# Strided attention and two split-precision MLPs on one core: the attention's end and the MLPs' beginning in another order, and the softmax's constant added on VectorE

## The chip, the cores and the metric

The kernel runs on one core of a Trainium2 chip. The metric is device time in microseconds (us); lower is better. TensorE multiplies matrices, VectorE and ScalarE work on tiles in SBUF and PSUM, GpSimd on tiles in SBUF, and SyncE issues the DMAs. In the profile they are called PE (PEld for the weight loads), DVE, ACT, POOL and SP.

## The reference

Attention over 2 x 8 heads of 576 tokens with 64 channels, each head with one of two masks, then an MLP with squared ReLU (512 to 2048 to 512), then four experts (512 to 1024 to 512) whose outputs are summed with normalised shares.

```python
scores = scale * np.matmul(q, k.transpose(0, 1, 3, 2))
scores = np.where(masks[None, :, :, :], scores, -1000000000.0)   # local: last 32; strided: same pos % 32
scores = scores - np.max(scores, axis=-1, keepdims=True)
attn = np.exp(scores)
attn = attn / (np.sum(attn, axis=-1, keepdims=True) + 1e-09)
x = np.matmul(attn, v)                       # then laid out as 1152 tokens x 512
h = np.maximum(x @ w_in, 0.0)
x = h * h @ w_out
for e in range(4):
    out += p[:, e:e + 1] * (np.maximum(x @ w1[e], 0.0) @ w2[e])
```

## The kernel before

**Attention.** It goes over eight pairs of heads n (0 to 7; 0, 1, 4, 5 are local, the others strided). For a pair TensorE computes the scores (L1065), VectorE adds the mask and takes the row extreme (`scores_max`, L725), ScalarE exponentiates block by block and accumulates the row sums in the same instruction (`exps`, L548), ScalarE adds 1e-9 to the sums (L554), VectorE takes the reciprocal (`recip`, L735), GpSimd multiplies (L493), TensorE transposes (L1085), VectorE copies the transposes out (`pT_copy`, L742), TensorE multiplies by v (`outputs`, L1111), and ScalarE or VectorE copies the result out (`att_out`). `warm_up` (L1119) are matmuls whose result nobody reads.

**MLPs.** A matrix product is split in two ways. Each float32 operand is split into a high and a low part, and three passes (L1122 to L1124) make one product. On top of it stands a seven-product scheme for 2 x 2 blocks (M1 to M7, computed in the order M1, M2, M6, M7, M4, M5, M3). Its input forms T1 to T4 are differences of blocks of x (`t_forms`, L770; `pair_forms` for the attention's end), S1 to S4 sums of weight blocks (`sums`, GpSimd). The high parts are made on ScalarE (`x_high`, `wa_high`, `wb_high`), the low parts on GpSimd (`x_low` L482, `wa_low` L442, `wb_low` L448). The combinations of the products are made by VectorE (`second_sum`, `third_sum`, `fourth_sum`, `c_block` L860) with a copy of M1 that ScalarE makes (`first_product`, L608). For the first MLP ScalarE takes the ReLU (`rectified`, L615), VectorE squares (`square`, L866), ScalarE writes `h_hi` (`h_high`, L622), VectorE writes `h_lo` (`h_low`, L873; L876 for the experts).

**Order.** The token halves and groups of 512 hidden units give 24 steps t. ORDER is A0, B0, A1, A2, B1, A3, B2, ... A7, B6, B7, A8, A9, B8, ...: "A t" computes the hidden block t (84 matmuls of the seven products), "B t" its share of the output (tiles of 12 matmuls). t below 8 is the first MLP; B's tiles alternate between two PSUM banks, and tile n waits until tile n - 2 is copied out (`y_copy` L600 on ScalarE for B0, `y_tile` L887 and L889 on VectorE from B1 on). Each engine runs its own list, written out by hand, strictly in that order; only semaphores tie the engines together. So the order in which an engine's code is written is the schedule. Block 0 starts inside the last pair of attention.

The waits of TensorE that matter below:

```python
elif k == M6:
    pe.wait_ge(s_m1, 2 * t + u + 1)
elif k == M7:
    pe.wait_ge(s_c, tile_count(t, C11, u))
...
if t == 0:
    pe.wait_ge(s_att, NP)
    pe.wait_ge(s_t[1], t_done(1, T4))
    pe.wait_ge(s_h_lo, tile_count(0, C21, 1))
```

In B0 the wait on `wb_lo` for the tile's own columns stands behind these, and the wait on all of block 0's `h_lo` stands at tile 4. In B8 the wait on all four `wb_lo` parts of the group stands behind the wait on `h_lo`.

Of the kernel before, what the change touches and what calls it, by code (L numbers as in the profile page):

```python
# [30 lines left out]
def attention_then_mlps(nc, qt, kt, v_near, v_far, wa, wb, probs, out):  # L31
# [57 lines left out]
    with ExitStack() as ctx:  # L89
# [71 lines left out]
        ssum = little("ssum", [P, 2, 2, 3, MAXB])  # L161
# [234 lines left out]
        def _(pool):  # L396
# [26 lines left out]
            nc.gpsimd.memset(ssum[:, :, :, :, :], 1.0).then_inc(s_stat_zero, 1)  # L423
# [62 lines left out]
            for n in range(NP):  # L486
# [3 lines left out]
                for h in range(2):  # L490
# [3 lines left out]
                        p_ap, p_ap, ssum[0:qw, n % 2, h, 2, 0:even].unsqueeze(2).to_broadcast([qw, even, kw]),  # L494
                        ALU.mult)
                    for i in range(even, nb):
# [3 lines left out]
                            p_ap, p_ap, ssum[0:qw_i, n % 2, h, 2, i:i + 1].to_broadcast([qw_i, kw_i]), ALU.mult)  # L500
# [21 lines left out]
            for kind, t in ORDER:  # L522
                s = t // 2
                if kind == "A" and t % 2 == 0 and 0 < t and s + 1 < SUBS:
                    sums(s + 1, S1, S3, S2, S4)
                if kind == "A" and t % 2 == 1:
# [3 lines left out]
                    if t == 1:  # L530
                        sums(1, S1, S3, S2, S4)
# [9 lines left out]
        def _(act):  # L541
            def exps(n, h, blocks):
                for i in blocks:
                    _, qw, _, kw, c0 = blocks_of(n)[i]
                    p_ap = prob[n % PROBS][0:qw, h, c0:c0 + kw]
                    if h == 0:
                        act.wait_ge(s_max, blocks_before(n) + i + 1)
                    ins = nc.scalar.activation(p_ap, p_ap, ACT.Exp, scale=-1.0, bias=smin[0:qw, n % 2, h, i:i + 1],  # L548
                                               accum_out=ssum[0:qw, n % 2, h, 0, i:i + 1])
                if i == len(blocks_of(n)) - 1:  # L550
                    ins.then_inc(s_exp, 1)
                    nb, qw = len(blocks_of(n)), blocks_of(n)[0][1]
# [63 lines left out]

            def h_high(t, q):
# [10 lines left out]
            act.wait_ge(s_stat_zero, 3)  # L628
# [17 lines left out]
            att_out(NP - 2)  # L646
            first_product(0)
            x_high(0, 3)
            x_high(0, 4)
# [23 lines left out]
            for k in (3, 4, 5, 6):  # L673
                x_high(1, k)
                y_copy(k + 1)
            for kind, t in ORDER[1:]:
                s = t // 2
                if kind == "B":
                    if t == BLOCKS1 - 2:
                        for k in range(FORMS):  # L680
                            x_high(2, k)
                    continue
                first_product(t)
                if t == 1:
                    for q in (C11, C21, C22, C12):
                        rectified(1, q)
                        if q != C12:
                            wa_high(1, 2 * q)
                        h_high(1, q)
                        if q != C12:  # L690
                            wa_high(1, 2 * q + 1)
                    wa_high(1, 6)
                    continue
# [3 lines left out]
                if t == BLOCKS1:  # L697
                    for k in range(FORMS):
                        x_high(3, k)
# [14 lines left out]
        def _(dve):  # L714
# [37 lines left out]
            def t_forms(i, *which):  # L752
                c = i % 2
                blocks, b12 = x_blocks(c)
                for k in which:
                    if i == 0:
                        dve.wait_ge(s_att, PAIRS)
                    else:
                        dve.wait_ge(s_y, y_tiles(BLOCKS1 - 4 + i) + (KT if k == T1 else 2 * KT))
# [10 lines left out]
                    nc.vector.tensor_tensor(t_form[:, c, k, :, :], a, b, ALU.subtract).then_inc(s_t[i], 1)  # L770

# [135 lines left out]
            dve.wait_ge(s_stat_zero, 3)  # L907
# [45 lines left out]
            for u in range(2):  # L953
                square(0, C22, u)
# [3 lines left out]
            for u in range(2):  # L958
                square(0, C12, u)
# [329 lines left out]
```

## Time and profile before

| | |
|---|---|
| three runs | 641.86, 642.80, 643.49 us (median 642.8) |
| the profiled execution | span 640.1 us, time 641.86 us |
| TensorE busy | 619.5 us (97%) |
| VectorE / ScalarE / GpSimd busy | 375.0 / 247.7 / 293.8 us |
| mean granted TensorE clock | 0.995 |

The profiled execution is the shortest of the three runs, 0.9 us below their median; between its span and its time lie 1.8 us. TensorE stands idle for 640.1 - 619.5 = 20.6 us of the span. A wait row names the releaser that the last wait instruction points to, which need not be the one that came last.

### The profile page before, as it was taken

What the parts mean: (1) busy time and instruction counts of PE and PEld (TensorE: products, weight loads), DVE (VectorE), ACT (ScalarE), POOL (GpSimd) and SP (SyncE); (2) the same over time, 40 slices, a digit from 0 to 9 for tenths busy, and PEclk for the clock granted to TensorE, in tenths of its full rate; (3) what the DMA queues carried; (4) which work ended last, traced back from release to release, by engine and by line L of the source; (5) the groups of instructions that cost most, each with busy time, mean ns of one, the idle gap of its engine ahead of it and who ended that gap; (6) DMA issues with size and microseconds to landing.
All of it is one profiled execution on the core that took longest, in us unless ns stands there. A gap on an engine that the chain in (4) does not pass through costs nothing.

```text
span 640.1 us, 11296 instructions
## 1 busy us (share of the span) xinstructions
PE 619.5 (97%) x4182; PEld 576.7 (90%) x4182; DVE 375.0 (59%) x980; ACT 247.7 (39%) x674; POOL 293.8 (46%) x249
## 2 busy tenths in 40 slices
PE   8879898999999999999999999999999999999998
PEld 7769897999999999989899899899899889889986
DVE  4876557585585586673564564564565465456452
ACT  6997655362362363461151151241241331232210
POOL 4987784255055058695065064074073173260200
PEclk9999998999999999999999999999999999999999
DMA  8440301012022012021011021011021022020012
GB/s 321 158 133 2 132 2 67 1 67 67 1 67 67 2 66 68 0 67 67 1 67 67 1 67 66 2 67 67 0 67 67 1 66 67 2 67 1 0 51 98
DMA packets 16486, 35.87 MB, mean 56 GB/s; under 512 B 2864, under 2 KB 3120, under 8 KB 16432
## 3 DMA queue, kind: packets, MB, share of 16 engines
q1 hardware_dynamic: 16432, 35.15, 16.4%
q8 instruction: 33, 0.54, 0.3%
q14 instruction: 21, 0.17, 0.1%
HBM read 32.79 MB, written 2.36 MB: 55 GB/s over the span
## 4 chain that ended last, share of the span: by engine, by line
PE 83%; DVE 7%; ACT 6%; issue 2%; POOL 2%; DVEq 0%; ACTq 0%; POOLq 0%
PE ps L1122 27%; PE ps L1124 26%; PE ps L1123 26%; ACT prob L548 3%; DVE h_lo L873 2%; DVE ps L860 1%; PE ps L1119 1%; DVE ps L866 1%; POOL xf_lo L482 1%; DVE prob L725 1%; PE ps L1065 1%; ACT xf_hi L595 1%; PE ps L1111 1%; ACT h_hi L622 1%; ACT wa_hi L572 1%
## 5 line engine op out<-in xcount | busy, mean ns | idle before, releaser
L1122 PE MATMUL ps<-xf_hi,wa_hi 128*128 128x288 f32 x672 | 200.4, 298 | 4.1 <-ACT m L608 3.7
L1123 PE MATMUL ps<-xf_lo,wa_hi 128*128 128x288 f32 x672 | 199.2, 296 | 0.0
L1124 PE MATMUL ps<-xf_hi,wa_lo 128*128 128x288 f32 x672 | 198.6, 296 | 0.0
L448 POOL TENSOR_TENSOR wb_lo<-raw_b,wb_hi 128x512 fp32r<-128x512 f32 x48 | 60.7, 1303 | 186.6 <-ACT wb_hi L581 186.6
L1122 PEld LDWEIGHTS ps<-xf_hi,wa_hi 128*128 128x128 f32 x672 | 127.0, 189 | 5.7 <-ACT wa_hi L572 3.5
L1123 PEld LDWEIGHTS ps<-xf_lo,wa_hi 128*128 128x128 f32 x672 | 126.9, 189 | 0.5
L1124 PEld LDWEIGHTS ps<-xf_hi,wa_lo 128*128 128x128 f32 x672 | 127.3, 189 | 0.0
L1122 PE MATMUL ps<-wb_hi,h_hi 128*128 128x512 f32 x288 | 112.3, 390 | 1.1 <-DVE h_lo L876 1.1
L1124 PE MATMUL ps<-wb_hi,h_lo 128*128 128x512 f32 x288 | 112.4, 390 | 0.0
L1123 PE MATMUL ps<-wb_lo,h_hi 128*128 128x512 f32 x288 | 112.4, 390 | 0.0
L903 DVE SCALAR_TENSOR_TENSOR y<-ps,p_norm,y 128x512 f32<-128x512 f32 (+1 forms) x64 | 47.4, 742 | 96.1 <-PE ps L1124 96.1
L625 ACT ACTIVATE h_hi<-ps 128x288 fp32r<-128x288 f32 x128 | 51.1, 410 | 106.6 <-DVE ps L860 106.6
L608 ACT ACTIVATE m<-ps 128x288 f32<-128x288 f32 x48 | 19.4, 412 | 182.9 <-PE ps L1124 182.9
L1122 PE MATMUL ps<-h_hi,wb_hi 128*128 128x288 f32 x256 | 76.5, 299 | 4.0 <-POOL wb_lo L448 1.6
L1124 PE MATMUL ps<-h_hi,wb_lo 128*128 128x288 f32 x256 | 75.5, 295 | 0.0
L1123 PE MATMUL ps<-h_lo,wb_hi 128*128 128x288 f32 x256 | 75.4, 295 | 0.0
L860 DVE TENSOR_TENSOR ps<-ps,u 128x288 f32<-128x288 f32 x144 | 66.9, 466 | 5.1 <-issue 0.4
L442 POOL TENSOR_TENSOR wa_lo<-raw_a,wa_hi 128x512 fp32r<-128x512 f32 x36 | 46.8, 1308 | 41.6 <-ACT wa_hi L572 41.6
L1122 PEld LDWEIGHTS ps<-wb_hi,h_hi 128*128 128x128 f32 x288 | 54.1, 188 | 12.1 <-DVE h_lo L876 1.3
L1124 PEld LDWEIGHTS ps<-wb_hi,h_lo 128*128 128x128 f32 x288 | 54.1, 188 | 11.4
L1123 PEld LDWEIGHTS ps<-wb_lo,h_hi 128*128 128x128 f32 x288 | 54.1, 188 | 10.9
L442 POOL TENSOR_TENSOR wa_lo<-s_form,wa_hi 128x512 fp32r<-128x512 f32 x48 | 61.1, 1293 | 5.2 <-ACT wa_hi L572 5.1
(77 smaller groups left out, 868.6 us busy)
## 6 DMA issues: line engine op xcount, KB each, us to landing
raw_a<-in_wa SPq DMA_DIRECT2D x48, 256.0 KB, 3.8
raw_b<-in_wb SPq DMA_DIRECT2D x24, 512.0 KB, 4.9
q_buf<-in_q SPq DMA_DIRECT2D x8, 288.0 KB, 4.7
k_buf<-in_k SPq DMA_DIRECT2D x8, 288.0 KB, 4.6
result<-y SPq DMA_DIRECT2D x8, 256.0 KB, 2.0
v_loc<-in_v_near SPq DMA_DIRECT2D x4, 384.0 KB, 4.6
v_str<-in_v_far SPq DMA_DIRECT2D x4, 320.0 KB, 5.5
result<-y SPq DMA_DIRECT2D x2, 128.0 KB, 1.8
```

The costliest lines, as they stand in the source:

```text
L442: nc.gpsimd.tensor_tensor(wa_lo[:, k, :, :], where[:, i, :, :], wa_hi[:, k, :, :].bitcast(F32), ALU.subtract).then_inc(s_wa_lo, 1)
L448: nc.gpsimd.tensor_tensor(wb_lo[:, :, cols], raw_b[:, :, cols], wb_hi[:, :, cols].bitcast(F32), ALU.subtract).then_inc(s_wb_lo, 1)
L482: nc.gpsimd.tensor_tensor(xf_lo[:, c, k, :, :], src, xf_hi[:, c, k, :, :].bitcast(F32), ALU.subtract).then_inc(s_xf_lo, 1)
L548: ins = nc.scalar.activation(p_ap, p_ap, ACT.Exp, scale=-1.0, bias=smin[0:qw, n % 2, h, i:i + 1], accum_out=ssum[0:qw, n % 2, h, 0, i:i + 1])
L608: nc.scalar.activation(m1[:, u, :], ps[:, bank(t, M1, u), 0:HT], ACT.Copy).then_inc(s_m1, 1)
L625: nc.scalar.activation(dst, src, ACT.Relu).then_inc(s_h_hi, 1)
L860: nc.vector.tensor_tensor(ps[:, hbank(t, q, u), 0:HT], ps[:, bank(t, k, u), 0:HT], other[:, u, :], ALU.add)\
L873: nc.vector.tensor_tensor(lo, ps[:, hbank(t, q, u), 0:HT], hi.bitcast(F32), ALU.subtract)\
L903: nc.vector.scalar_tensor_tensor(out=out_acc[:, i, d], in0=src, scalar=p_norm[:, i, e:e + 1], in1=out_acc[:, i, d], op0=ALU.mult, op1=ALU. ...
L1122: nc.tensor.matmul(dst, a_hi, b_hi, start=first, stop=False)
L1123: nc.tensor.matmul(dst, a_hi, b_lo, start=False, stop=False)
L1124: return nc.tensor.matmul(dst, a_lo, b_hi, start=False, stop=last)
```

## The change

**Softmax.** The 16 ScalarE instructions that add 1e-9 go. The accumulated sum and a constant 1e-9 now lie side by side (two more small memsets on GpSimd at the start), and VectorE sums the two with a `tensor_reduce` ahead of each reciprocal.

**End of attention.** TensorE computes M2 of block 0 in two halves with the outputs of pair 6 and the next transposes between them. ScalarE copies M1 and makes one x form ahead of `att_out` of pair 6.

**Block 0.** ScalarE takes over the squares of C22 and C12, and its list around them is reordered. **Block 1.** ScalarE copies M1 of block 2 ahead of the last `h_high`. **B blocks.** `y_tile` 1 moves between the two halves of C22. **Transition to the experts.** The forms T2 to T4 of sets 2 and 3 are made in halves inside B6 and B7, the high parts of set 3 are interleaved with `h_high` of block 8, and GpSimd makes the sums of group 5 behind `wb_low` of group 4.

```diff
-            return {T1: 1, T2: 2, T3: 3, T4: 4}[k]
+            return {T1: 1, T2: 5, T3: 6, T4: 7}[k]
...
-                if kind == "A" and t % 2 == 0 and 0 < t and s + 1 < SUBS:
+                if kind == "A" and t % 2 == 0 and t not in (0, BLOCKS1) and s + 1 < SUBS:
                     sums(s + 1, S1, S3, S2, S4)
                 if kind == "A" and t % 2 == 1:
                     if t > 1:
                         for d in range(KT):
                             wb_low(s, d)
-                    if t == 1:
-                        sums(1, S1, S3, S2, S4)
+                    if t in (1, BLOCKS1 + 1):
+                        sums(s + 1, S1, S3, S2, S4)
...
-                                               accum_out=ssum[0:qw, n % 2, h, 0, i:i + 1])
+                                               accum_out=ssum[0:qw, n % 2, h, i, 0:1])
                 if i == len(blocks_of(n)) - 1:
                     ins.then_inc(s_exp, 1)
-                    nb, qw = len(blocks_of(n)), blocks_of(n)[0][1]
-                    act.wait_ge(s_exp, 2 * n + h + 1)
-                    nc.scalar.activation(ssum[0:qw, n % 2, h, 1, 0:nb], ssum[0:qw, n % 2, h, 0, 0:nb], ACT.Copy,
-                                         bias=1e-9).then_inc(s_sum, 1)
...
+            def squared(t, q):
+                for u in range(2):
+                    act.wait_ge(s_relu, tile_count(t, q, u))
+                    nc.scalar.activation(ps[:, hbank(t, q, u), 0:HT], relu[:, u, :], ACT.Square).then_inc(s_sq, 1)
...
-            att_out(NP - 2)
             first_product(0)
             x_high(0, 3)
+            att_out(NP - 2)
...
             x_high(1, 0)
             rectified(0, C22)
+            squared(0, C22)
+            h_high(0, C22)
             y_copy(0)
             x_high(1, 1)
-            h_high(0, C22)
+            rectified(0, C12)
+            squared(0, C12)
+            h_high(0, C12)
             y_copy(1)
-            rectified(0, C12)
             x_high(1, 2)
-            y_copy(2)
-            h_high(0, C12)
-            y_copy(3)
...
+                    rectified(1, C12)
+                    first_product(2)
+                    h_high(1, C12)
                     wa_high(1, 6)
...
             def recip(n, h):
                 nb, qw = len(blocks_of(n)), blocks_of(n)[0][1]
+                dve.wait_ge(s_exp, 2 * n + h + 1)
+                nc.vector.tensor_reduce(srec[0:qw, n % 2, h, 0, 0:nb], ssum[0:qw, n % 2, h, 0:nb, :], AX.X, ALU.add)\
+                    .then_inc(s_sum, 1)
                 dve.wait_ge(s_sum, 2 * n + h + 1)
...
+            def half_forms(i, kt):
...
+                dve.wait_ge(s_y, y_tiles(BLOCKS1 - 4 + i) + KT + 2 * (kt + 1))
+                for k in (T2, T3, T4):
...
+                    nc.vector.tensor_tensor(t_form[:, c, k, kt, :], a[:, kt, :], b[:, kt, :], ALU.subtract)\
+                        .then_inc(s_t[i], 1)
...
-                            if i == 0:
-                                for u in range(2):
-                                    h_low(follows[1], C22, u)
-                                    c_block(follows[1], C12, u)
+                            if i < 2:
+                                h_low(follows[1], C22, i)
+                                c_block(follows[1], C12, i)
...
+                        if t >= BLOCKS1 - 2 and i == KT - 1:
+                            t_forms(t - BLOCKS1 + 4, T1)
+                        if t >= BLOCKS1 - 2 and i in (KT + 1, KT + 3):
+                            half_forms(t - BLOCKS1 + 4, (i - KT) // 2)
...
                 if n == NP - 1:
-                    product(0, M2)
+                    product(0, M2, [0])
...
             prob_transposes(NP - 1, 0)
+            product(0, M2, [1])
             product(0, M6, [0])
```

Three places in the engines' order. ScalarE at the end of block 1, where `relu`, `h_hi`, `wa_hi` and `m` are the outputs of `rectified`, `h_high`, `wa_high` and `first_product`; before:

```order
L572 ACTIVATE wa_hi<-s_form 128x512
L615 ACTIVATE relu<-ps 128x288 x2
L572 ACTIVATE wa_hi<-raw_a 128x512
L622 ACTIVATE h_hi<-ps 128x288 x2
L572 ACTIVATE wa_hi<-s_form 128x512
L615 ACTIVATE relu<-ps 128x288 x2
L622 ACTIVATE h_hi<-ps 128x288 x2
L572 ACTIVATE wa_hi<-s_form 128x512
L608 ACTIVATE m_62<-ps 128x288 x2
```

and after, where the copy of M1 (`m`) stands ahead of the last `h_hi`:

```order
L573 ACTIVATE wa_hi<-s_form 128x512
L616 ACTIVATE relu<-ps 128x288 x2
L573 ACTIVATE wa_hi<-raw_a 128x512
L628 ACTIVATE h_hi<-ps 128x288 x2
L573 ACTIVATE wa_hi<-s_form 128x512
L616 ACTIVATE relu<-ps 128x288 x2
L609 ACTIVATE m_62<-ps 128x288 x2
L628 ACTIVATE h_hi<-ps 128x288 x2
L573 ACTIVATE wa_hi<-s_form 128x512
```

The copy moved forward past one pair of `h_hi` and one `wa_hi`.

VectorE in B1, where `y` is `y_tile`, `h_lo` and `ps<-ps,u` are `h_low` and `c_block` of the block computed ahead of it; before:

```order
L887 COPY y<-ps 128x288
L873 TENSOR_TENSOR h_lo<-ps,h_hi 128x288
L860 TENSOR_TENSOR ps<-ps,u_63 128x288
L873 TENSOR_TENSOR h_lo<-ps,h_hi 128x288
L860 TENSOR_TENSOR ps<-ps,u_63 128x288
L887 COPY y<-ps 128x288
L866 SCALAR_TENSOR_TENSOR ps<-ps,relu 128x288 x2
L887 COPY y<-ps 128x288
L873 TENSOR_TENSOR h_lo<-ps,h_hi 128x288 x2
```

and after:

```order
L929 COPY y<-ps 128x288
L915 TENSOR_TENSOR h_lo<-ps,h_hi 128x288
L902 TENSOR_TENSOR ps<-ps,u_63 128x288
L929 COPY y<-ps 128x288
L915 TENSOR_TENSOR h_lo<-ps,h_hi 128x288
L902 TENSOR_TENSOR ps<-ps,u_63 128x288
L908 SCALAR_TENSOR_TENSOR ps<-ps,relu 128x288 x2
L929 COPY y<-ps 128x288
L915 TENSOR_TENSOR h_lo<-ps,h_hi 128x288 x2
```

The second `y` moved forward past one `h_lo` and one `c_block`; nothing else moved.

GpSimd at the transition, where `xf_lo` are the low parts of x sets 2 and 3, `s_form` the sums of group 5 and `wb_lo` the low parts of group 4; before:

```order
L482 TENSOR_TENSOR xf_lo<-t_form,xf_hi 128x576 x4
L482 TENSOR_TENSOR xf_lo<-y,xf_hi 128x576
L458 TENSOR_TENSOR s_form<-raw_a 128x512
L460 TENSOR_TENSOR s_form<-raw_a 128x512
L464 TENSOR_TENSOR s_form<-s_form,raw_a 128x512
L468 TENSOR_TENSOR s_form<-raw_a,s_form 128x512
L448 TENSOR_TENSOR wb_lo<-raw_b,wb_hi 128x4x128 x4
L442 TENSOR_TENSOR wa_lo<-raw_a,wa_hi 128x512 x2
```

and after:

```order
L487 TENSOR_TENSOR xf_lo<-y,xf_hi 128x576 x3
L487 TENSOR_TENSOR xf_lo<-t_form,xf_hi 128x576 x4
L487 TENSOR_TENSOR xf_lo<-y,xf_hi 128x576
L453 TENSOR_TENSOR wb_lo<-raw_b,wb_hi 128x4x128 x4
L463 TENSOR_TENSOR s_form<-raw_a 128x512
L465 TENSOR_TENSOR s_form<-raw_a 128x512
L469 TENSOR_TENSOR s_form<-s_form,raw_a 128x512
L473 TENSOR_TENSOR s_form<-raw_a,s_form 128x512
L447 TENSOR_TENSOR wa_lo<-raw_a,wa_hi 128x512 x2
```

The four `wb_lo` moved ahead of the four `s_form`.

## Rows read from the trace of the kernel before

**Rows 1.** Windows: length, PE, PEld, DVE, ACT, POOL busy (instructions), clock, DMA share, GB/s.
```profile
20.00:45.00 25.00, 20.74 (x257) 17.96 (x258) 20.29 (x125) 24.72 (x115) 22.39 (x22) 1.00 0.56 173
...
46.70:50.10 3.40, 3.40 (x32) 3.18 (x29) 1.19 (x5) 2.84 (x12) 3.07 (x3) 0.50 0.02 5
84.00:94.00 10.00, 10.00 (x77) 10.00 (x77) 6.51 (x16) 4.85 (x11) 8.65 (x8) 1.00 0.00 1
101.30:104.70 3.40, 3.40 (x16) 3.40 (x16) 1.65 (x5) 0.77 (x2) 0.67 (x1) 0.50 0.42 133
264.00:290.00 26.00, 24.53 (x161) 22.80 (x160) 19.41 (x45) 14.75 (x33) 24.49 (x20) 1.00 0.13 42
290.00:600.00 310.00, 310.00 (x1817) 281.29 (x1816) 166.67 (x346) 85.52 (x196) 115.89 (x92) 1.00 0.13 42
```

**Rows 2.** Waits of TensorE, whole run: waiter, named releaser, us in total, times, longest.
```profile
PE ps L1122 <- ACT m L608: 3.7, 2, 3.1
...
PE ps L1119 <- DVE probT L742: 2.1, 1, 2.1
...
PE ps L1122 <- POOL wb_lo L448: 1.6, 1, 1.6
PE ps L1122 <- DVE y L889: 1.2, 5, 0.3
PE ps L1122 <- DVE h_lo L876: 1.1, 1, 1.1
```

**Rows 3.** TensorE in order of time: start, length, instruction, idle before it and named releaser.
```profile
69.14 0.37 PE L1122 MATMUL ps<-h_hi,wb_hi 128*128 128x288 f32 x1 [1.59 <-POOL wb_lo L448]
...
76.66 0.40 PE L1122 MATMUL ps<-h_hi,wb_hi 128*128 128x288 f32 x1 [0.96 <-DVE h_lo L873]
...
97.36 0.29 PE L1122 MATMUL ps<-xf_hi,wa_hi 128*128 128x288 f32 x1
...
101.06 0.37 PE L1122 MATMUL ps<-xf_hi,wa_hi 128*128 128x288 f32 x1 [3.15 <-ACT m L608]
...
139.49 0.30 PE L1122 MATMUL ps<-h_hi,wb_hi 128*128 128x288 f32 x1
...
140.31 0.40 PE L1122 MATMUL ps<-h_hi,wb_hi 128*128 128x288 f32 x1 [0.26 <-DVE y L889]
...
281.77 0.29 PE L1122 MATMUL ps<-xf_hi,wa_hi 128*128 128x288 f32 x1
...
283.42 0.47 PE L1122 MATMUL ps<-wb_hi,h_hi 128*128 128x512 f32 x1 [1.09 <-DVE h_lo L876]
```

**Rows 4.** The small operations of lines 554 and 807: ns min/median/max, starts.
```profile
L554 ACT ACTIVATE ssum<-ssum x16: 206/208/209, 9.8 to 53.0; 96x6 f32<-96x6 f32 x8, 126x5 f32<-126x5 f32 x8
...
L807 DVE TENSOR_REDUCE p_sum<-p_raw x1: 180/180/180, 124.4 to 124.4; 128x9 f32<-128x36 f32 x1
```

**Rows 5.** VectorE in order of time, places of the first two MLP blocks and before.
```profile
41.89 0.18 DVE L735 RECIPROCAL ssum<-ssum 96x6 f32<-96x6 f32 x1 [1.36 <-ACT ssum L554]
...
68.48 0.45 DVE L873 TENSOR_TENSOR h_lo<-ps,h_hi 128x288 fp32r<-128x288 f32 x1
...
139.80 0.45 DVE L889 TENSOR_TENSOR y<-ps,y 128x288 f32<-128x288 f32 x1
```

**Rows 6.** ScalarE in order of time, blocks 0 and 1 of the first MLP.
```profile
69.46 0.41 ACT L615 ACTIVATE relu<-ps 128x288 f32<-128x288 f32 x1 [0.45 <-DVE ps L860]
...
71.00 0.41 ACT L600 ACTIVATE y<-ps 128x288 f32<-128x288 f32 x1 [1.13 <-PE ps L1124]
...
98.39 0.70 ACT L615 ACTIVATE relu<-ps 128x288 f32<-128x288 f32 x2
...
100.51 0.70 ACT L608 ACTIVATE m<-ps 128x288 f32<-128x288 f32 x2
```

**Rows 7.** GpSimd in order of time, ahead of the first expert block's output.
```profile
278.12 5.04 POOL L448 TENSOR_TENSOR wb_lo<-raw_b,wb_hi 128x512 fp32r<-128x512 f32 x4
```

**Rows 8.** Line 770, differences of two SBUF tiles: ns min/median/max, starts.
```profile
L770 DVE TENSOR_TENSOR t_form<-y x5: 719/1067/1394, 46.8 to 264.3; 128x576 f32<-128x576 f32 x5
```

More of the change, by code:

```diff
@@ L663, in _ @@
             rectified(0, C22)
+            squared(0, C22)
+            h_high(0, C22)
             y_copy(0)
             x_high(1, 1)
-            h_high(0, C22)
+            rectified(0, C12)
+            squared(0, C12)
+            h_high(0, C12)
             y_copy(1)
-            rectified(0, C12)
             x_high(1, 2)
-            y_copy(2)
-            h_high(0, C12)
-            y_copy(3)
-            for k in (3, 4, 5, 6):
-                x_high(1, k)
-                y_copy(k + 1)
+            for k in (2, 3, 4, 5):
+                y_copy(k)
+                x_high(1, k + 1)
+            y_copy(6)
+            y_copy(7)
             for kind, t in ORDER[1:]:
@@ L681, in _ @@
                             x_high(2, k)
+                    if t == BLOCKS1 - 1:
+                        x_high(3, 0)
                     continue
-                first_product(t)
+                if t != 2:
+                    first_product(t)
                 if t == 1:
-                    for q in (C11, C21, C22, C12):
+                    for q in (C11, C21, C22):
                         rectified(1, q)
-                        if q != C12:
-                            wa_high(1, 2 * q)
+                        wa_high(1, 2 * q)
                         h_high(1, q)
-                        if q != C12:
-                            wa_high(1, 2 * q + 1)
+                        wa_high(1, 2 * q + 1)
+                    rectified(1, C12)
+                    first_product(2)
+                    h_high(1, C12)
                     wa_high(1, 6)
+                    continue
+                if t == BLOCKS1:
+                    x_high(3, 1)
+                    x_high(3, 2)
+                    h_high(t, C11)
+                    x_high(3, 3)
+                    h_high(t, C21)
+                    x_high(3, 4)
+                    x_high(3, 5)
+                    h_high(t, C22)
+                    x_high(3, 6)
+                    h_high(t, C12)
                     continue
@@ L770, in t_forms @@
                     nc.vector.tensor_tensor(t_form[:, c, k, :, :], a, b, ALU.subtract).then_inc(s_t[i], 1)
+            def half_forms(i, kt):
+                c = i % 2
+                blocks, b12 = x_blocks(c)
+                dve.wait_ge(s_y, y_tiles(BLOCKS1 - 4 + i) + KT + 2 * (kt + 1))
+                for k in (T2, T3, T4):
+                    if k == T2:
+                        dve.wait_ge(s_t[i], 1)
+                        a, b = blocks[B22], t_form[:, c, T1, :, :]
+                    elif k == T3:
+                        a, b = blocks[B22], b12
+                    else:
+                        dve.wait_ge(s_t[i], 3 * kt + 2)
+                        a, b = blocks[B21], t_form[:, c, T2, :, :]
+                    nc.vector.tensor_tensor(t_form[:, c, k, kt, :], a[:, kt, :], b[:, kt, :], ALU.subtract)\
+                        .then_inc(s_t[i], 1)
             def pair_t1(n):
@@ L971, in _ @@
                         second_sum(t, u)
-                    if t == BLOCKS1:
-                        t_forms(3, T3, T4)
                     if moe1(t):
```

36 lines of the change are left out of this document (11 added, 25 removed).

## Prediction

> **What bounds the kernel now.** I read the windows first. From 290 to 600 us TensorE is busy for all 310.00 us; in 264 to 290 us it is busy for 24.53 of 26.00 us [rows 1]. So the experts' steady part has nothing to give, and the change, which touches only what lies before about 290 us, can only work on TensorE's gaps there. The list of TensorE's waits names them: 3.7 us for the copy of M1 (3.1 of it in one wait), 1.6 for `wb_lo`, 1.2 in five waits for `y`, 1.1 for `h_lo` (L876), and 2.1 once for `probT` in attention [rows 2]. Then I went to each place in TensorE's order of time. Three passes of a 128x288 product stand 0.40 us apart where nothing is waited for (77 matmuls in 10.00 us, some records missing [rows 1]), so what a wait costs is the start after it less the start before it, less 0.40. This slip is larger than the idle time in the row. It is 101.06 - 97.36 - 0.40 = 3.30 us for M6 of block 2, 140.31 - 139.49 - 0.40 = 0.42 for tile 3 of a B block, 283.42 - 281.77 - 0.40 = 1.25 at the start of B8 [rows 3].
>
> Two names mislead. At 69.14 the row names `wb_lo` [rows 3], but the wait that counts is that on `h_lo` of C21 ahead of it: VectorE wrote it at 68.48 and ended at 68.93 [rows 5]. At 283.42 the row names `h_lo` [rows 3], but four `wb_lo` run from 278.12 for 5.04 us, to 283.16 [rows 7]. I take these two as the releasers, because TensorE starts 0.2 to 0.3 us behind them.
>
> The clock is the last view. TensorE was granted half of its full clock (1.2 for 2.4 GHz) from 46.7 to 50.1 us and from 101.3 to 104.7, full clock in the other windows read [rows 1]. The second fall comes just as the 3.15 us wait ends at 101.06; in it TensorE did 16 matmuls in 3.40 us against 3.40 / 0.133 = 25.5 at full clock, which is 9.5 x 0.133 = 1.3 us lost, and 1.5 by the ratio of the clocks less the first few passes. I take 1.4.
>
> **The change, part by part.** *Constant on VectorE.* It removes 16 ScalarE instructions of 0.208 us [rows 4], 3.3 us. In 20 to 45 us ScalarE is busy for 24.72 of 25.00 us, VectorE for 20.29, GpSimd for 22.39 [rows 1]. The early ones gain nothing, since `att_out` of the first pairs waits for TensorE's outputs. From pair 3 on ScalarE leads until the reciprocal at 41.89, for which VectorE stood idle for 1.36 us [rows 5]. Five of the removed instructions lie in that stretch: 5 x 0.21 = 1.05 us. The added `tensor_reduce` isn't in the trace in this shape; the nearest row is that of line 807 with 0.18 us [rows 4], and about 0.07 for the wait of the reciprocal on it, so I take 0.25 each. Ahead of the reciprocal it stands in for ScalarE's instruction. But VectorE works in order, and behind the reduce of pair 6 waits a `pT_copy` for which TensorE waits: +0.25. Bounds for a reduce: nothing (the wait hidden) and 0.5 (a reduce as long as VectorE's 128x288 work, 0.45 [rows 5]). Sum -0.8, bounds -1.3 and +0.5. The two memsets end before the first scores arrive. This costs nothing unless the first ones grow by microseconds.
>
> *M2 in halves, M1's copy earlier.* No matmul is added. M6 waited 3.7 - 3.1 = 0.6 us for M1's copy [rows 2], which stood behind `att_out` of pair 6; now the copy comes first and half of M2 covers the rest: -0.6, bounds -0.9 and 0. GpSimd gets its x forms some 2 us earlier. That hides, but buys nothing: B0's start is set by VectorE's `h_lo` of C21, and VectorE's list up to it is untouched. So the wait at 69.14 stays, only shifted.
>
> *Squares on ScalarE in block 0.* ScalarE's list around the `y_copy` of 71.00 changes, before which it stood idle for 1.13 us [rows 6]. I lay its new list out from the second ReLU of C22 at 69.46, with 0.31 from start to start for two 128x288 of the same kind (a pair takes 0.70, one 0.41 [rows 6]): squares at 69.8 and 70.1, `h_hi` at 70.4 and 70.7, `y_copy` 0 at 71.0, x form at 71.3, ReLUs of C12 at 71.9 and 72.7 (behind VectorE's two `c_block`), squares 73.0 and 73.3, `h_hi` 73.6 and 73.9, `y_copy` 1 at 74.2 to 74.6. Tile 4's wait for `h_lo`, 0.96 idle at 76.66 [rows 3] and 1.1 as slip, goes. In its place tile 3, which would start at 69.14 + 3 x 1.6 = 73.9, waits for `y_copy` 1 until 74.7: 0.8. Net -0.3, bounds -1.1 (the squares quicker) and +0.5 (each square dearer by 0.2). If `Square` needed another activation table, loads would be added; the built list has one table load, as before.
>
> *M1's copy of block 2.* Before, the two ReLUs of C12 stand at 98.39 and the two copies at 100.51, with TensorE released at 101.06 by the first of them, 0.55 after its start [rows 3, 6]. Now the copies follow the ReLUs: first one at 98.39 + 2 x 0.31 = 99.0, TensorE at 99.55, 1.5 us earlier. Behind the copies wait `h_hi` and `h_lo` of C12 and then the `c_block` for which M7 waits; it comes at about 101.25 and M7 would want to start at 99.55 + 1.6 = 101.15, so 0.25 of it is given back. -1.25, bounds -1.5 and -0.8. What is left of the gap is 1.8 us. The wait of 1.59 at 69.14 [rows 3] is as long and lies between dense matmuls as well, and the clock did not fall behind it. So I count the fall as gone: -1.4, bound 0.
>
> *`y_tile` 1 earlier in B1 to B6.* Before, the copy at 139.80 ended at 140.25 and TensorE went on at 140.31 [rows 3, 5]. Moved ahead of one `h_low` and one `c_block`, it ends some 0.85 us earlier, and the slip of 0.42 goes. But `c_block` of the second half comes 0.37 later, and ReLU, square and `y_tile` 2 follow it; tile 4 then waits about 0.14. Six blocks x 0.28 = -1.7; bounds -2.5 (six whole slips) and -0.6.
>
> *Transition.* Without the two `t_forms` in the middle of block 8, VectorE no longer holds up M3 of block 8 and M1 of block 9: idle 24.53 against 26.00 us [rows 1] is 1.47, of which 1.09 is the wait at 283.42 [rows 3], so 0.4 here, some 0.7 as slip. GpSimd makes `wb_lo` ahead of four sums of 1.3 us, and the slip of 1.25 at 283.42 goes. -1.95. What is queued behind: the sums then end about where `wa_lo` began before, 283.1, and block 10 has five tiles of B8 to wait for. The half forms cost VectorE more in B6 and B7. Line 770 with two tiles of x took 0.72 to 1.39 us for 576 columns [rows 8]. Three halves at 0.4 to 0.75 and their waits are 1.4 to 2.5 us between `y_tile` 5 and 6; up to 2.3 the tiles hide it, above that tile 0 of B7 waits: bounds -1.95 and -1.3.
>
> On those 1.39 us the Trainium skill, "SBUF — State Buffer", on the shared port pair, says that a VectorE instruction with two SBUF inputs contends with a GpSimd instruction that reads SBUF, and the second to issue blocks until the first has finished. By that rule a half form beside GpSimd's 1.3 us work would wait for it whole: three forms near 3 us, a stall of some 0.6 at B7's tile 0. The trace bears out that the same form takes twice the time at some places, not which of the two waits.
>
> Sum: 0.8 + 0.6 + 0.3 + 1.25 + 1.4 + 1.7 + 1.95 = 8.0 us. On the profiled execution's own 641.86 that gives 633.9. It was the shortest of the three, 0.9 below the median, so a median of the changed kernel may stand as much above its best; I take 634.4.
>
> **Rivals.** (1) *The clock still falls behind the remaining 1.8 us.* For it: in attention it fell after a shorter wait, the 2.1 us for `probT` [rows 2], though among short matmuls. 634.4 + 1.4 = 635.8. (2) *Attention gains more.* VectorE and ScalarE being shorter, the wait of 2.1 us for `probT` [rows 2] shrinks to about 1.3, and the fall at 46.7 [rows 1] goes: 634.4 - 1.5 = 632.9. (3) *VectorE becomes attention's bound and ScalarE's new list stalls B0.* VectorE has 25.00 - 20.29 = 4.7 us of idle time, but in small waits on TensorE; the reduces take 9 x 0.25 = 2.3 of it. Then the first and third terms are lost: 635.5 to 637. (4) *Slower.* A single mechanism: the reduce and the wait on it. There are 16, in order, ahead of `pT_copy` and `scores_max`. If each cost p, attention would grow by 16 x (p - 0.25) once VectorE's slack is used, and the whole becomes slower than 642.8 + 1.9 where that exceeds 10.3 us, p = 0.9: 645 and more. Against it: 0.18 us for a larger one [rows 4]. (5) *The waits only move:* the B blocks wait at tile 4, B8 for something else behind `wb_lo`, B7 at tile 0. Then 1.7 + 1.25 + 0.7 are lost: 638, and with (3) 641.
>
> **How the numbers follow.** Forecast 0.45, (1) 0.15, (2) 0.17, (3) 0.12, (4) 0.02, (5) 0.09 (0.04 of it together with (3), up to no change). The range 631.3 to 638.3 holds the forecast with most of its bounds, (1), (2) and (3). A difference of 0.3% (1.9 us) is about what a measurement of this kernel can tell from no change. Faster 0.93, the same 0.05, slower 0.02.
>
> **What would show it.** In the profile of the changed kernel: the wait for M1's copy near 100 us about 1.6 instead of 3.15, and full clock behind it; no wait of 0.3 at tile 3 of the B blocks, perhaps one below 0.2 at tile 4; no wait of 1.1 at B8's start; a wait near 67 us still there, still named `wb_lo`; a wait for `y` of ScalarE in B0. Wrong would be: a reduce above 0.3 us, the wait for `probT` grown, a table load among the squares, a new half-clock stretch.

## The result, and the profile after

The changed kernel takes 634.87 us (median of four executions, 634.16 to 636.45) against 642.33 us for the kernel before on the same chip (641.78 to 643.49). The ratio is 0.9885, 95% interval 0.9859 to 0.9911: 1.15% faster. The forecast was 634.4 with a range of 631.3 to 638.3. The profiled execution took 634.17 us, 0.7 below the median, and its mean clock was 1.000; two of the four had 0.997 (635.57 and 636.45 us).

The page of the kernel after, its span and the busy time of each engine:

```profile
span 632.4 us, 11306 instructions
...
PE 615.5 (97%) x4182; PEld 573.2 (91%) x4182; DVE 382.0 (60%) x998; ACT 245.4 (39%) x662; POOL 294.6 (47%) x251
```

TensorE is busy for 4.0 us less than before with the same matmuls, most of it from the two stretches at half clock [rows 1], which this execution doesn't have; it is idle for 16.9 us where it was idle for 20.6. Windows of the kernel after, the same stretches as in [rows 1] and then whole blocks from TensorE's first matmul to the first of the next (M7 of block 0 to A1, A1 and A2, B6 and B7, A8 and A9):

```profile
20.00:45.00 25.00, 21.81 (x267) 18.83 (x265) 22.90 (x138) 24.36 (x114) 23.57 (x23) 1.00 0.58 173
...
264.00:290.00 26.00, 26.00 (x155) 23.62 (x154) 16.04 (x37) 11.29 (x26) 22.32 (x18) 1.00 0.20 61
290.00:600.00 310.00, 310.00 (x1836) 282.33 (x1836) 168.06 (x351) 89.02 (x204) 117.79 (x94) 1.00 0.12 40
...
57.28:79.29 22.01, 19.70 (x149) 19.29 (x145) 10.08 (x28) 15.09 (x37) 18.72 (x15) 1.00 0.29 97
79.29:103.97 24.68, 23.05 (x170) 22.45 (x169) 18.72 (x47) 14.24 (x36) 13.72 (x12) 1.00 0.13 43
224.91:253.39 28.48, 26.09 (x195) 25.57 (x193) 23.30 (x40) 11.54 (x24) 21.76 (x15) 1.00 0.15 53
253.39:275.78 22.39, 22.39 (x170) 22.39 (x169) 17.14 (x42) 11.94 (x28) 16.50 (x13) 1.00 0.08 19
```

The same blocks in the kernel before:

```profile
83.16:110.65 27.49, 24.34 (x171) 23.96 (x170) 19.11 (x47) 14.42 (x36) 16.62 (x14) 0.94 0.12 40
60.88:83.16 22.28, 19.73 (x148) 19.29 (x145) 11.95 (x32) 14.09 (x34) 17.58 (x14) 1.00 0.29 95
...
258.93:283.42 24.49, 23.02 (x171) 22.40 (x169) 18.65 (x44) 13.54 (x31) 20.13 (x16) 1.00 0.01 1
...
232.90:258.93 26.03, 25.77 (x194) 25.51 (x193) 17.22 (x34) 11.19 (x23) 19.69 (x14) 1.00 0.16 58
```

Read in pairs they give the balance: A1 and A2 gain 27.49 - 24.68 = 2.81 us, A8 and A9 gain 24.49 - 22.39 = 2.10, block 0 from M7 on gains 22.28 - 22.01 = 0.27, and B6 and B7 **lose** 28.48 - 26.03 = 2.45. The experts' steady part is busy for its whole 310.00 us in both. M7 of block 0 starts at 57.28 instead of 60.88 (3.60, of which 0.25 is an earlier start of this execution and no work of the change, as experiment 3 shows), and B1 to B5 gain 0.22 to 0.29 each (1.3).

TensorE's waits after, which answer to [rows 2]:

```profile
PE ps L1152 <- DVE y L931: 2.3, 1, 2.3
...
PE ps L1152 <- ACT m L609: 1.6, 1, 1.6
PE ps L1152 <- issue: 1.6, 1, 1.6
...
PE ps L1149 <- DVE probT L767: 1.1, 1, 1.1
PE ps L1152 <- ACT y L601: 0.7, 1, 0.7
```

The longest wait for `m` went from 3.1 to 1.6, that for `probT` from 2.1 to 1.1; the `h_lo` L876 wait of 1.1 and the five for `y` (L889) are gone. New are 0.7 for ScalarE's `y`, which the prediction foresaw at 0.8, and the first row, 2.3 us once, ended at 240.59, ahead of B7's tile 0. What VectorE did then, in order of time, with GpSimd below:

```profile
232.62 1.70 DVE L795 TENSOR_TENSOR t_form<-y 128x576 f32<-128x576 f32 x1
...
235.50 1.55 DVE L811 TENSOR_TENSOR t_form<-y,t_form 128x288 f32<-128x288 f32 x1
236.96 1.54 DVE L811 TENSOR_TENSOR t_form<-y 128x288 f32<-128x288 f32 x1
238.43 1.65 DVE L811 TENSOR_TENSOR t_form<-y,t_form 128x288 f32<-128x288 f32 x1
240.00 0.81 DVE L931 TENSOR_TENSOR y<-ps,y 128x288 f32<-128x288 f32 x2
240.84 0.46 DVE L811 TENSOR_TENSOR t_form<-y,t_form 128x288 f32<-128x288 f32 x1
```

```profile
233.64 1.83 POOL L447 TENSOR_TENSOR wa_lo<-raw_a,wa_hi 128x512 fp32r<-128x512 f32 x1
235.43 2.76 POOL L447 TENSOR_TENSOR wa_lo<-s_form,wa_hi 128x512 fp32r<-128x512 f32 x2
238.15 1.61 POOL L487 TENSOR_TENSOR xf_lo<-y,xf_hi 128x576 fp32r<-128x576 f32 x1
241.61 1.74 POOL L487 TENSOR_TENSOR xf_lo<-y,xf_hi 128x576 fp32r<-128x576 f32 x1 [1.84 <-ACT xf_hi L596]
```

The first three half forms of a set take 1.5 to 1.65 us each beside GpSimd's differences; the fourth, of the same shape, takes 0.46 in a stretch in which GpSimd is idle (239.8 to 241.6). T1 of the same set, a whole form of 576 columns beside GpSimd (232.62), takes 1.70: hardly more than a half. The `y_tile` behind the three comes at 240.00, and TensorE starts at 240.59.

### The profile page after: what moved, and what is told of

Same layout as the page of the kernel before. It is cut to its first block, busy times and chain, and to the rows that moved or that the text cites. A ratio compares the mean times of both kernels' runs of the same rounds, so it can differ in the third digit from the quotient of the medians.

```text
span 632.4 us, 11306 instructions
## 1 busy us (share of the span) xinstructions
PE 615.5 (97%) x4182; PEld 573.2 (91%) x4182; DVE 382.0 (60%) x998; ACT 245.4 (39%) x662; POOL 294.6 (47%) x251
## 4 chain that ended last, share of the span: by engine, by line
PE 93%; DVE 5%; issue 1%; ACT 1%; DVEq 0%; POOL 0%; POOLq 0%; ACTq 0%
PE ps L1152 30%; PE ps L1154 29%; PE ps L1153 29%; PE ps L1149 2%; DVE prob L747 2%; PE ps L1095 2%; PE ps L1141 1%; PE ps L1115 1%; DVE probT L767 1%; DVE t_form L811 1%; DVE h_lo L915 0%; DVE ps L902 0%; ACT h_hi L628 0%; ACT relu L616 0%; DVE ps L908 0%
```

## The experiments

Each kernel ran beside the kernel before on its chip. Line numbers shift by a few between them.

**1. Is it the half forms at all?** The changed kernel, with T2 to T4 whole and at the places that they had before.

```diff
-                        if t >= BLOCKS1 - 2 and i == KT - 1:
-                            t_forms(t - BLOCKS1 + 4, T1)
-                        if t >= BLOCKS1 - 2 and i in (KT + 1, KT + 3):
-                            half_forms(t - BLOCKS1 + 4, (i - KT) // 2)
+                        if t == BLOCKS1 - 2 and i == KT - 1:
+                            t_forms(2, T1)
+                        if t == BLOCKS1 - 1 and i == 0:
+                            t_forms(2, T3)
...
+                    if t == BLOCKS1:
+                        t_forms(3, T3, T4)
```

> The changed kernel with the x forms of the transition made whole and at their places of before (T1, T3, T4, T2 in B6 and B7, two in block 8). Theory: the 2.3 us wait of TensorE at the start of B7, which the changed kernel has and the old one had not, comes from the half forms, each of which took 1.5 us beside GpSimd. Then the wait goes, B6 and B7 take 26.0 us again instead of 28.5, some 0.5 us of the gain of block 8 is lost, and the span falls by about 2 us, to 630.4; time near 632.2. Rival: the wait comes from the new place of y tile 1 or of the high parts of set 3; then the wait stays and the span stays near 632.4 or rises by 0.5.

Measured: 631.79 us (631.6 to 632.31) against 641.83, ratio 0.9836 (0.9813 to 0.986). B6 and B7 in a window:

```profile
225.62:251.52 25.90, 25.85 (x195) 25.55 (x193) 18.45 (x34) 11.88 (x24) 20.22 (x15) 1.00 0.16 58
```

25.90 us against 28.48: the wait for `y` is gone and the half forms, where they stand, cost the change 2.6 us. The run changes the size and the place of the forms together; whole forms at the place of the halves were not run. A8 and A9 still take 22.39 us, though the two whole forms stand in block 8 again.

**2. Is it GpSimd beside them?** The changed kernel with its half forms, but GpSimd's low parts of group 4 for 8 of every 256 columns only (it leaves out the rest of these low parts, so the first expert block works with stale ones).

```diff
-                nc.gpsimd.tensor_tensor(wa_lo[:, k, :, :], where[:, i, :, :], wa_hi[:, k, :, :].bitcast(F32),
+                w = 8 if s == BLOCKS1 // 2 else GF // 2
+                nc.gpsimd.tensor_tensor(wa_lo[:, k, :, 0:w], where[:, i, :, 0:w], wa_hi[:, k, :, 0:w].bitcast(F32),
```

> The changed kernel, in which GpSimd makes the low parts of the weights of group 4 for 8 columns of 256 only (the rest is left out, so the first expert block's low parts are stale). The half forms stay. Theory: a half form waits for the GpSimd instruction that it meets, whole. With GpSimd's seven instructions at the end of B6 short, the half forms take 0.45 us instead of 1.5 and TensorE's wait at B7 of 2.3 us goes; span near 630.0, if the low parts of set 2 that come earlier then don't take their place as partners (if they do, the half forms of B6 still show 1.4 us where a 128x576 GpSimd instruction runs). Rival: half forms take 1.5 us of themselves in this place; then they stay at 1.5 and the span at 632.4.

Measured: 631.72 us (631.27 to 632.29), ratio 0.9834 (0.981 to 0.9858). The same VectorE instructions, then GpSimd's one difference near them:

```profile
235.61 0.65 DVE L812 TENSOR_TENSOR t_form<-y,t_form 128x288 f32<-128x288 f32 x1
236.18 0.45 DVE L812 TENSOR_TENSOR t_form<-y 128x288 f32<-128x288 f32 x1
236.55 0.45 DVE L812 TENSOR_TENSOR t_form<-y,t_form 128x288 f32<-128x288 f32 x1
```

```profile
234.50 1.44 POOL L488 TENSOR_TENSOR xf_lo<-y,xf_hi 128x576 fp32r<-128x576 f32 x1 [0.35 <-ACT xf_hi L597]
```

Nothing was changed on VectorE, and 1.55, 1.54, 1.65 became 0.65, 0.45, 0.45; the 0.65 is the one that began before GpSimd's instruction ended at 235.94. The wait for `y` is gone. So what a half form costs here is set by GpSimd beside it. The Trainium skill, "SBUF — State Buffer", section "SBUF: two separate sides", says that VectorE with two SBUF inputs and GpSimd reading SBUF take a shared port pair in turn, each for a whole instruction. The trace agrees for VectorE: in the changed kernel the three long half forms end at 237.05, 238.50 and 240.08, and GpSimd's instructions at about 236.8, 238.2 and 239.76, each 0.25 to 0.32 us earlier. On GpSimd's side it shows less than a whole turn: beside a half form its instructions are 0.12 to 0.3 us longer (1.38 for 1.26, 1.61 and 1.74 for 1.44), not the form's 0.45.

**3. The parts by themselves**, each put alone into the kernel before.

*The constant:* the `tensor_reduce` in `recip` and the two memsets, with ScalarE's 16 instructions taken out.

> The kernel before with the constant added on VectorE, and nothing else of the change. By the prediction's first term the reciprocal of each pair starts about as much earlier as the ScalarE instruction took (0.21 us) less the VectorE sum (0.16 us, from the trace after), and ScalarE loses 16 instructions of 0.21 us, two of which lie on the path to the last pair's work: TensorE's M7 of block 0 starts 0.8 us earlier than the 60.88 us of before (60.1), the stretches behind it stay as before, and the time is 0.8 us less, 641.0. The theory that this part alone removes the fall of TensorE's clock at the attention's end: no stretch at 1.2 GHz between 44 and 52 us, M7 at 58.6, time 639.5. If neither the sums nor the list of ScalarE are on the path here: M7 at 60.9, 641.8.

*The order at attention's end:*

```diff
-            att_out(NP - 2)
             first_product(0)
             x_high(0, 3)
+            att_out(NP - 2)
...
-                    product(0, M2)
+                    product(0, M2, [0])
...
+            product(0, M2, [1])
             product(0, M6, [0])
```

> The kernel before with only the order at the attention's end: M2 of block 0 in two halves, and ScalarE's copy of M1 and one x form ahead of the output copy of pair 6. By the prediction's second term M7 of block 0 starts 0.6 us earlier (60.3) and the time is 0.6 us less, 641.2. The theory that the half of M2 fills the wait that let the clock fall: the wait of 2.1 us there shrinks to about 1.1 us, no stretch at 1.2 GHz between 44 and 52 us, M7 at 58.8 and 639.7. If only the two parts together remove the fall, this kernel and the one with the constant alone both keep it.

*The copy of M1 of block 2* (`first_product(2)` behind the last `rectified` of block 1, nothing else):

> The old kernel with only the copy of M1 of block 2 moved ahead of the last h_high of block 1. Theory: the wait of 3.15 us near 101 falls to 1.6, M7 waits at most 0.3 behind it, and the fall of the clock behind it goes in most executions: from B0's end to B1's start 24.7 us instead of 27.5. Time 2.6 us below the old kernel where the clock falls there in the old one and not in this one, 1.3 where it makes no difference. Rival: the gap of 1.8 us still brings the clock down; then 1.3 us and the half-clock stretch stays.

*`y_tile` 1* between the halves of C22:

> The kernel before with only the second y_tile of the B blocks moved ahead of the second half of C22. By the prediction the wait of 0.22 to 0.29 us at the third tile goes from each of B1 to B6: TensorE from A1's start to A8's start takes 1.7 us less than the 175.77 us of before, and the time is 640.1. The rival that the half of C22 moved behind the copy is late for what needs it: a wait of 0.2 us or more appears ahead of A blocks or of B's first tiles and the gain is under half, 641 or more.

*The sums of group 5* behind `wb_low` of group 4:

> The old kernel with only the sums of group 5 moved behind the low parts of the output weights of group 4 on GpSimd. Theory: the wait at the start of B8 (1.09 us idle, 1.25 as slip), whose row names h_lo, is one for wb_lo; then it goes and blocks 8 and 9 take 23.2 us instead of 24.5; time 1.25 us below the old kernel. Rival: the row is right and h_lo is what is late; then nothing changes.

| alone | us (executions) | ratio to before (95%) | predicted gain | gain by medians | in the trace |
|---|---|---|---|---|---|
| constant | 639.83 (10) | 0.9975 (0.9963 to 0.9988) | 0.8 | 1.95 | wait for `probT` 2.13 to 1.05, no fall of the clock behind it |
| attention's end | 640.84 (10) | 0.9986 (0.9971 to 1.0) | 0.6 | 0.9 | wait for `probT` stays 2.13, the clock falls for longer, M7 at 61.83 |
| copy of M1 | 638.75 (8) | 0.9956 (0.9938 to 0.9975) | 2.65 | 3.1 | A1 and A2 24.67 |
| `y_tile` 1 | 639.76 (8) | 0.9968 (0.9949 to 0.9987) | 1.7 | 2.0 | A1 to A8 174.12 for 175.77 |
| sums of group 5 | 640.42 (10) | 0.9979 (0.9963 to 0.9995) | 1.25 of 1.95 | 1.4 | A8 and A9 23.23 for 24.49 |

The windows of the last three, A1 and A2, A1 to A7, A8 and A9:

```profile
82.88:107.55 24.67, 23.04 (x170) 22.45 (x169) 18.65 (x47) 14.24 (x36) 15.26 (x13) 1.00 0.13 45
```

```profile
82.65:256.77 174.12, 170.79 (x1262) 169.10 (x1261) 117.61 (x274) 74.16 (x174) 83.28 (x64) 0.99 0.13 43
```

```profile
258.96:282.19 23.23, 22.86 (x171) 22.46 (x170) 17.46 (x41) 12.73 (x29) 17.54 (x14) 1.00 0.07 14
```

These gains are small against the scatter. That of attention's end isn't shown by its time, since the interval reaches 1.0; its profile is that of the slowest of ten executions (642.78 us at a mean clock of 0.992, the other nine 639.59 to 641.04), and M7 starts at 61.83 in it, not at the 60.3 expected. The other four intervals lie below 1.

The five gains add up to 9.4 us. The whole change without its stall (experiment 1) brings 10.0, so 0.6 is left for what was not run alone: the squares on ScalarE and ScalarE's interleaving at the transition. The sum is a rough one, since the first two parts both act on the same fall of the clock.

From TensorE's first instruction behind the wait for `probT` to M7 of block 0, in the kernel before, with the constant alone, after, and with attention's end alone:

```profile
44.82:60.88 16.06, 15.41 (x144) 14.38 (x144) 10.16 (x34) 12.77 (x47) 11.94 (x14) 0.89 0.01 2
```

```profile
44.27:58.78 14.51, 13.85 (x144) 12.87 (x144) 11.40 (x38) 12.00 (x43) 12.00 (x14) 1.00 0.01 2
```

```profile
43.46:57.28 13.82, 13.72 (x144) 12.87 (x144) 11.53 (x38) 12.33 (x43) 12.38 (x14) 1.00 0.01 2
```

```profile
45.30:61.83 16.53, 16.53 (x144) 15.68 (x145) 10.38 (x34) 13.13 (x47) 13.61 (x15) 0.80 0.01 2
```

The constant alone takes 1.08 us off the wait and 16.06 - 14.51 = 1.55 off the stretch, all of it the clock (0.89 to 1.00). The order at attention's end takes another 14.51 - 13.82 = 0.69 off, its predicted 0.6; alone it leaves the wait as it was, and the clock falls all the same, in this execution for longer (0.80 for 0.89).

Where M7 starts in a profile also depends on when the execution got going. One and the same group of score matmuls, in the same four kernels:

```profile
19.54 0.35 PE L1065 MATMUL ps<-k_buf,q_buf 64*72 64x72 f32 x4
```

```profile
20.10 0.35 PE L1067 MATMUL ps<-k_buf,q_buf 64*72 64x72 f32 x4
```

```profile
19.29 0.35 PE L1095 MATMUL ps<-k_buf,q_buf 64*72 64x72 f32 x4
```

```profile
20.01 0.35 PE L1065 MATMUL ps<-k_buf,q_buf 64*72 64x72 f32 x4
```

The kernel of experiment 1, whose attention is that of the changed kernel, has it at 20.07 and M7 at 58.05, so the 0.8 us between it and the changed kernel's profile is scatter. From this group to M7 it is 41.34 us before, 38.68 with the constant alone, 37.99 after (37.98 in experiment 1). The constant thus gives 2.66, of which 1.55 is the clock and 1.11 its own; the order gives 0.69; and 0.25 of the 3.60 at M7 is the start.

**4. Where the spread of the changed kernel comes from.** The changed kernel once more, beside the last kernels of experiment 5.

> The changed kernel itself, on the same chip as the two others, so that these are compared with it as well as with the kernel before. 634.2 us where TensorE's clock never falls, about 1.4 us more where it falls once, a median of 634.2 to 635.6. The difference to the kernels with whole forms should be 2.4 to 2.6 us plus what the two edits of block 0 and block 1 bring.

Measured: 636.23 us (635.95 to 636.53) against 641.62, ratio 0.9918 (0.9903 to 0.9933), 1.4 us above the first result. B6 and B7, and a part of B7:

```profile
225.31:255.33 30.02, 27.62 (x194) 27.10 (x193) 22.18 (x40) 11.54 (x24) 21.70 (x15) 0.94 0.14 50
241.40:244.80 3.40, 3.40 (x16) 3.40 (x15) 1.51 (x4) 3.40 (x6) 2.79 (x2) 0.51 0.52 193
```

Here the clock fell to half (1.2 GHz) right behind the 2.3 us wait at B7, and the two blocks take 30.02 us instead of 28.48. By the mean clocks such a fall was there in all four executions on this chip (0.997 each) and in two of the four of the first result (635.57 and 636.45; the other two, 634.16 and 634.17, had 1.000); the place is seen in the profiled one alone. So the stall costs 2.6 us, and 1.5 more where the clock answers.

**5. Can the rest of the waits go?** First both `h_lo` of C21 ahead of the `c_block` of C22 in block 0, on top of experiment 1:

```diff
             for u in range(2):
                 h_low(0, C21, u)
+            for u in range(2):
                 c_block(0, C22, u)
```

> The changed kernel with the transition's forms whole and at the places of before, as in the first experiment (631.8 us, span 630.5), and in block 0 both h_lo of C21 ahead of the first c_block of C22 on VectorE. If the idle time ahead of B0 (1.6 us at 65.5) is the wait for h_lo of C21's second half, B0 starts about 0.5 us earlier (the c_block that stood between them takes 0.45 to 0.5), its later waits on block 0's chain grow by no more than 0.3, and the time is 631.3 to 631.6. If that idle time is the wait for wb_lo, which the profile of before names, B0's start stays 8.2 us behind M7 as it is now, what follows is later by nothing or by 0.2, and the time is 631.8 to 632.0. A gain of more than 0.8 is not expected by either.

Measured: 632.12 us (631.87 to 632.17), ratio 0.9847 (0.9825 to 0.9869). B0 starts 7.75 us behind M7 (65.85 after 58.10) for 8.25 in the changed kernel: 0.5 earlier, so the wait that both profiles call `wb_lo` or "issue" was for `h_lo`, as the prediction read it. By A1 half of this is given back, and in the time nothing is to be seen: 632.12 where 631.3 to 631.6 was expected, and 631.79 without the edit, on another chip. Next the copy of M1 earlier still:

```diff
+                    rectified(1, C22)
+                    first_product(2)
+                    h_high(1, C22)
+                    wa_high(1, 4)
                     rectified(1, C12)
-                    first_product(2)
+                    wa_high(1, 5)
                     h_high(1, C12)
```

> The kernel with the transition's forms whole and both h_lo of C21 first, and the copy of M1 of block 2 still earlier: ahead of h_high of C22 in block 1, where ScalarE waits 0.23 us for VectorE anyway, with wa_high 5 moved behind the last rectified. M1 of block 2 has been complete since about 91.1 us there, and TensorE waits 1.62 us for the copy at 94.6. If the copy's place in ScalarE's list is all that this wait is made of, it goes: TensorE from A1's start to B1's takes 23.2 us (24.68 before), every block behind it starts 1.5 us earlier, and the time is 630.4 to 630.7. If VectorE's c_block of C11 (97.45 there) is late next, M7 of block 2 waits 0.3 us or more and the gain is 1.2 or less. No gain if something else than the copy held M6.

Measured: 633.56 us (633.55 to 633.57), ratio 0.9876 (0.9862 to 0.9891), where the kernel without this edit had 0.9847 (0.9825 to 0.9869) on another chip: no gain, and 1.4 us longer in A1 and A2. TensorE in order of time, and A1 and A2 in a window:

```profile
97.95 0.37 PE L1165 MATMUL ps<-xf_hi,wa_hi 128*128 128x288 f32 x1 [1.78 <-DVE ps L906]
```

```profile
79.82:105.94 26.12, 24.34 (x170) 23.95 (x169) 18.83 (x47) 14.25 (x36) 13.85 (x12) 0.93 0.13 41
```

The expected gain of 1.5 us did not come. The wait for the copy went, but the branch with a late `c_block` held: M7 waited 1.78 us for it, far above the 0.3 that was named as the least, and the clock fell behind it (26.12 for 24.68; all four executions have 0.997). The copy had covered a second wait that was as long. Then VectorE's list of block 0, the squares of C21 ahead of the last pair's forms and the fourth sum behind `c_block` C22:

> The same with VectorE's list of block 0 in another order: the squares of C21 ahead of the x forms of the last pair, and the fourth sum behind the c_block of C22. By the trace h_lo of C21 then ends 0.5 to 0.8 us earlier and B0 starts 7.0 to 7.3 us behind M7 of block 0 (7.75 in the kernel without it), while the fourth sum falls into 1.4 us in which VectorE waited. The wait at B0's tile 4 (0.97 us) stays or grows to 1.2, since it ends with the chain of C22 and C12 and that becomes only 0.5 shorter. M7 to A1 takes 21.2 to 21.4 us (21.74 without), the time is 0.4 to 0.5 less: 629.9 to 630.3. If the time to B0's start is bound by something else (the x forms, wb_lo), B0 starts where it did.

Measured: 632.35 us (631.53 to 632.93), ratio 0.9856 (0.9839 to 0.9872). M7 of block 0 to A1 takes 21.23 us, as expected (78.75 - 57.52; 21.74 in the kernel of the first edit), B0 starts 7.23 behind M7. The time missed its 629.9 to 630.3, because the wait at M7 of block 2 is still there (1.76 us) and A1 and A2 take 26.12 us as before. Last, the `c_block` that M7 waited for, taken ahead of the squares and `h_lo` of C12, which it doesn't need:

```diff
                             for u in range(2):
                                 h_low(t, q, u)
+                            if t == 1 and q == C22:
+                                for u in range(2):
+                                    c_block(2, C11, u)
```

> The kernel with whole forms at the transition, block 0's VectorE list reordered and the copy of M1 of block 2 ahead of h_high of C22, and now VectorE's c_block of C11 of block 2 ahead of the squares and h_lo of block 1's C12. In the kernel before this step TensorE waited 1.78 us at M7 of block 2 for this c_block, which stood behind them and started at 97.4, while VectorE was idle for 0.36 us at 95.1. If VectorE's list is all that is left of this wait, it goes, TensorE from A1's start to B1's takes 22.9 to 23.1 us (26.12 with the wait and the clock's fall behind it, 24.68 with a wait and no fall), no stretch at 1.2 GHz follows there, and the time is 629.4 to 630.2. If second_sum or a later sum of block 2 is late instead, a wait of 0.3 to 1.5 us appears at M4 or M5 of block 2 and the time is 630.2 to 631.5.

Measured: 630.11 us (629.54 to 630.51) against 641.90, ratio 0.9815 (0.9801 to 0.9828). A1 and A2 in a window, and the waits of the MLP blocks:

```profile
79.20:102.30 23.10, 22.83 (x171) 22.43 (x169) 18.34 (x46) 14.06 (x35) 13.50 (x11) 1.00 0.10 33
```

```profile
PE ps L1169 <- ACT y L601: 1.0, 1, 1.0
PE ps L1169 <- POOL wb_lo L453: 0.6, 1, 0.6
PE ps L1169 <- DVE u L866: 0.3, 1, 0.3
```

23.10 us for 24.68, full clock, and 0.3 us left for a later sum. The wait before B0 is down to 0.6. This kernel lies 11.8 us below the kernel before, and about 4.5 below the changed one (0.9885 - 0.9815 = 0.7% of 642, each ratio against the kernel before beside it; 6.6 by the ratio of experiment 4).

## Why the prediction was right, and where it wasn't

The time came out 0.5 us above the forecast, but that is luck: two errors cancel. M7 of block 0 came 2.2 us earlier than the terms for attention say, and B7's stall took 2.45 that were in no term. Each of the other terms came out within 0.4 us.

- **Constant, -0.8.** The mechanism held: the reduce takes 0.15 us (against 0.18 to 0.25 taken), and the wait for `probT` shrank. Alone the constant gives 1.11 us of its own for the term's 0.8, and 1.55 by the clock. The term left out that the clock would no longer fall. That was rival (2), taken at 0.17: the wait went to 1.1 us (1.3 foreseen) and the fall was gone in the profile. The constant alone does it in the profiled execution; four of its ten executions have the mean clock of the kernel before.
- **M2 in halves, -0.6.** 0.69 in the trace, on top of the constant; the 0.6 us for which M6 waited for M1's copy are gone. With these two terms, 0.25 of M7's 3.60 us is the start of the execution.
- **Squares, -0.3.** 22.28 to 22.01, 0.27; a wait of 0.72 for ScalarE's `y` stands where 0.8 was forecast, and B0's first wait is as long as before (1.58). A `Square` took 0.41 us, as the ReLU, and ScalarE's list has one table load, as before.
- **M1's copy and the clock behind it, -1.25 and -1.4.** 2.81 for 2.65, and 2.82 with this part alone. The wait that is left is 1.6 (1.8 forecast) and the clock held in the profile. That was a bet: experiment 5 shows it fall behind a wait of 1.78 us at nearly the same place.
- **`y_tile`, -1.7.** 0.22 to 0.29 us a block against 0.28, 1.3 in B1 to B5; what it gives in B6 is hidden by the stall. Alone 1.65.
- **Transition, -1.95.** Two errors here. The gain in A8 and A9 was 2.10, of which 1.26 are the sums of group 5 (1.25 forecast). But the reason for the other 0.8 was wrong: the prediction gave it to the two `t_forms` leaving the middle of block 8, and experiment 1 puts them back there without a loss. What remains of the change in these blocks is ScalarE's interleaving of `x_high` and `h_high`; it was not run alone, so the cause of this 0.84 stays open. The failed step is "three halves at 0.4 to 0.75": they take 1.54 to 1.65 beside GpSimd, 4.5 us from 235.50 to the `y_tile` at 240.00 against the 2.3 that the tiles hide, a stall of 2.3. The bound was half of the slowest whole form [rows 8], 1.39 / 2, as if the price went with the columns. It goes with GpSimd's instruction, whose length doesn't change when the form is cut. The sentence on the skill's rule foresaw a stall at this very tile, at 0.6; it counted three times 1 us where a form waits for most of a GpSimd instruction and then runs its own 0.45. Rival (5) named a wait of B7 at tile 0 too; of its waits this one alone came. And one sign named for being wrong came true: a new half-clock stretch, behind this stall, in experiment 4.

## What to carry to other kernels

Here a VectorE instruction with two SBUF inputs, cut in half beside a busy GpSimd, took nearly as long as the whole one (1.54 to 1.65 us for 1.70), so two halves that both meet it cost nearly twice as much. Cut it where GpSimd is idle or its instructions are short, as in experiment 2. When a wait of TensorE is removed, look at once for the next one behind it on the other engine's list: it may be as long, and in block 2 the move paid only when both were moved. A wait of about 2 us between matmuls cost another 1.5 here where the clock fell behind it, so a small gain that shortens such a wait may pay more than its own length. Before two profiles are compared by where something starts, compare an early instruction that the change doesn't touch: it differed by up to 0.8 us between executions.

## What the runs showed of the hardware

- A 128x288 `tensor_tensor` from two SBUF tiles took 0.45 us with GpSimd idle and 1.54 to 1.65 beside its 128x512 and 128x576 differences. A whole one, 128x576, took 1.70 beside them. GpSimd's own were stretched as well: 1.38 us each at 235.43 (two in 2.76), against 1.26 (four in 5.04 [rows 7]), and 1.83 beside the whole form.
- The times of the kernel before come in rough steps by the mean clock. Of 23 executions of the kernel before, beside the constant, attention's end, `y_tile` and the first kernel of experiment 5, three at a mean clock of 1.000 took 638.9 to 639.1 us, two at 0.997 took 640.5, sixteen at 0.995 took 641.1 to 642.0, two at 0.992 took 643.5: 0.6 to 2.4 us from step to step. With the constant alone, six of ten stood at 0.997 (639.3 to 639.8) and four at 0.995 (640.1 to 640.4), a step of about half a us. So the mean clock alone doesn't give the time.
- The clock fell behind waits of 2.1, 2.3 and 3.1 us in most executions, but not in all, and behind one of 1.78 us; behind waits of 1.6 us at nearly the same place the profiles show none. In the profile with the constant alone it did not fall behind a wait of 1.05 us in attention, where it fell behind 2.13. What decides it stays open.
